# Wider joins of solved blocks, a router written as rows, and more filler products in the routing

## The chip, the cores and the metric

The kernel runs on one core of a Trainium2 chip. The metric is the device time of one execution in microseconds. All data is fp32. The engines are TensorE (PE: matmul, and its weight loads, PEld), VectorE (DVE), ScalarE (ACT), GpSimd (POOL) and SyncE (SP, which here only issues DMAs).

## What is computed

A recurrence over 768 steps for 4 x 8 heads of width 40, and two mixtures of experts on its output, each of which sends a token to one of 8 experts.

```python
for t in range(S):                                   # S = 768
    y[:, :, t] = einsum('bhd,bhde->bhe', rt, state)
    Sa = einsum('bhde,bhe->bhd', state, at)
    state = state * wt[:, :, None, :] - einsum('bhd,bhe->bhde', Sa, bt) \
            + einsum('bhd,bhe->bhde', vt, kt)
x = y as (3072 tokens, 320)
# layer 1: e = argmax(x @ w_gate); out = softmax weight * sigmoid(x @ w_output_gate)[e] * relu(x @ w1[e]) @ w2[e]
# layer 2: the same without the output gate, on layer 1's output, with a capacity of 768 tokens per expert
```

w1[e] is 320 x 1024 and w2[e] 1024 x 320.

## The kernel before

**The recurrence.** Time is cut into chunks of 64 steps (C) and the work into 12 sets (NK): a set k is 128 steps (two chunks, c = 0 and 1) of 16 heads, so 32 pieces, 16 on each side h of the partitions (rows 0 to 63 and 64 to 127). Within a chunk the steps depend on each other through a lower triangle of 64 x 64 (a Gram matrix of a and b, `G_b`), which has to be solved: T = (1 - G)^-1. It is solved in blocks. Four diagonal blocks of 16 (BLK) are solved by DVE in `solve`, all heads at once, on rows that go out to DRAM and come back in another layout (`send_g`, `fetch_g`; `send_t`, `fetch_t`, `fetch_d`). Then PE joins them: two blocks of 16 to one of 32 by `join_first` (G times T, to `A_sb`) and `join_second` (D_nat^T times A_sb, to T_T through `t16_out`), for both halves m of the chunk; then two blocks of 32 to 64 by `quotient` and `corner`.

**The order.** Each engine has its program, and all are built from one loop over slots j = -3 to 12, with two halves c = 0, 1 each. In slot j the chain of the state runs for set j (`right_side`, `state_natural`, `solved`, `state`, `inner`, `outputs`), the solving for set j + 1 and `grams_b` for set j + 2. On PE the half c = 1 has `right_side`, `grams_b(j+2)`, `state_natural`, `natural`, `outputs`, `join_first(j+1)`, `turn_y`, `solved`, `state`, `grams_k`, `join_second(j+1)`, `inner`, `quotient(j+1)`. The half c = 0 has `right_side`, `grams_k`, `corner`, `state_natural`, `outputs`, `natural`, `solved`, `state`, `inner`. DVE's `m_out` (line 1277) masks what `inner` made and so ends each half; after the one of c = 1 DVE does `solve(j+2)`, on which POOL's `scale_a` and `scale_run` wait, and on these PE's next `grams_b` (line 856).

**Lines.** A product is one call of `mm`; in the trace an fp32 product is two matmuls and two weight loads. `join_first` is line 909, `join_second` 924, `quotient` 938, `corner` 955, `right_side` 969, `state_natural` 986, `grams_k` 875, `solved` 997 and 1005, `inner` 1037 and 1041, `outputs` 1054 and 1062, `turn_y` 1073. ACT's copies all have line 665: `gb_out` (G_b), `ga_out` (A_sb), `t16_out` (T_T), `u_out` (ZV). POOL: `scale_a` 575, `scale_run` 582, `mask_gk` 589.

**The second router.** In slot 2 ACT's queue issues one DMA (line 761) that writes the second router's weights, 320 x 8, transposed into DRAM (`wr_dram`). Before the experts begin, SP's queue spreads them over all partitions (`wr_next`, line 540).

**The routing**, once per layer: a chain of small DVE operations on [128, 24 x 8]; PE counts tokens with two products (1128), then does WARM products of 128 x 128 by 512 whose result nobody reads (1132), then 24 products (1136) that sort tokens and gates into 31 tiles, in four lots, each after one of four DVE operations of line 1419 (`place_set`). After it DVE hands the tokens to POOL, which gathers rows by indirect DMA.

**The experts**: 31 tiles of 128 tokens per layer. PE: `up(i+1)` (1160, 1167), `turn_x(i+2)` (1147), `down(i)` (1179). ACT and DVE: relu (816, 1444). DVE: `result` (1451) and, in the first layer, `next_logits`, a multiplication of `wr_next` by the tile's rows (1458) and a sum (1462). DVE's order per tile is relu of i + 1, result of i, logits of i; POOL stores the tile (646) after its logits. `lg_parts` holds partial logits of the first router between `x_out` on ACT and `lg_sum` on DVE.

## Time and profile before

| | us |
|---|---|
| median of 3 runs | 1289.96 (1289.43 to 1297.5) |
| the profiled execution | 1287.04 |
| its span | 1285.3 |

| engine | busy us | share |
|---|---|---|
| PE | 1097.9 | 85% |
| PE weight loads | 949.7 | 74% |
| DVE | 558.7 | 43% |
| ACT | 396.4 | 31% |
| POOL | 302.4 | 24% |

The busy times come from the page, which also has the chain of work that ended last, followed back from the last instruction. The mean granted clock of PE over the whole span is 0.876 of full speed. In what follows a "stretch" is a piece of time between two given points, in us from the start of the span. "issue" is time in which an engine waited for nothing that the profile shows.

### The profile page before, as it was taken

Reading aid. Unit: us, or ns where it says so; the run is one execution under the profiler, and the core shown is the slowest. Engines: PE = TensorE matmul, PEld = TensorE weight load, DVE = VectorE, ACT = ScalarE, POOL = GpSimd, SP = SyncE. Lnnn points to the kernel's source line nnn. Section 1 sums busy time; section 2 is a strip of 40 time slices with the busy share of each in tenths; the row PEclk is TensorE's granted clock in tenths of the full one; section 3 lists DMA queues with packets and bytes.
Section 4 is the critical chain, followed back from the end, with each engine's and each line's share of the span. In section 5 each row is a group of like instructions: output and inputs, shape, how many; then the busy total and the mean of one; then the engine's idle time right before and its main releaser. Section 6 shows DMA issues by size and latency. Waiting matters only on the chain.

```text
span 1285.3 us, 41335 instructions
## 1 busy us (share of the span) xinstructions
PE 1097.9 (85%) x18328; PEld 949.7 (74%) x18328; DVE 558.7 (43%) x864; ACT 396.4 (31%) x550; POOL 302.4 (24%) x253
## 2 busy tenths in 40 slices
PE   1189894888898889986899999999569999997997
PEld 0188784777888878885788888888448888876885
DVE  6635363364536443416176777767650111110111
ACT  0033332333333334331333333333004333323330
POOL 5440443043034213000112122121201212121111
PEclk8557997896888689777799999999868999998999
DMA  3333439343334333216024224333300331443000
GB/s 84 93 96 84 101 88 68 78 95 81 95 74 110 81 88 74 56 40 199 18 74 146 66 77 129 98 115 103 87 7 29 123 107 61 141 139 112 21 11 1
DMA packets 143115, 107.64 MB, mean 84 GB/s; under 512 B 91553, under 2 KB 120233, under 8 KB 142813
## 3 DMA queue, kind: packets, MB, share of 16 engines
q1 hardware_dynamic: 130560, 84.99, 25.0%
q0 software_dynamic: 6016, 16.05, 3.9%
q10 hardware_dynamic: 6364, 3.96, 2.0%
q8 instruction: 148, 2.42, 0.8%
q14 instruction: 27, 0.21, 0.1%
HBM read 87.51 MB, written 22.09 MB: 85 GB/s over the span
## 4 chain that ended last, share of the span: by engine, by line
PE 76%; DVE 8%; issue 7%; POOL 3%; DMA 3%; ACT 2%; SPq 1%; ACTq 0%; POOLq 0%; DVEq 0%
PE pair L1179 19%; PE pair L1160 17%; PE pair L1167 5%; PE pair L986 4%; PE bank L1054 3%; PE pair L1147 2%; PE pair L875 2%; PE pair L1073 2%; POOL AG L575 2%; PE bank L969 2%; PE bank L1062 2%; PE pair L892 2%; PE pair L924 2%; PE bank L1136 2%; PE pair L909 2%
## 5 line engine op out<-in xcount | busy, mean ns | idle before, releaser
L1179 PE MATMUL pair<-abk_own,H_nat 128*128 x992 | 277.7, 433 | 1.7 <-DVE S_nat L1451 1.7
L1160 PEld LDWEIGHTS pair<-H_nat,rvm 128*128 128x128 f32 x1984 | 238.3, 197 | 23.0 <-ACT H_nat L665 14.2
L1160 PE MATMUL pair<-H_nat,rvm 128*128 128x128 f32 x1984 | 239.6, 281 | 11.9 <-ACT H_nat L665 11.9
L1179 PEld LDWEIGHTS pair<-abk_own,H_nat 128*128 128x128 f32 x992 | 183.9, 190 | 71.3 <-issue 2.7
L665 ACT ACTIVATE rvm<-ring_own 128x2560 f32 x62 | 145.0, 2339 | 149.5 <-issue 86.0
L816 ACT ACTIVATE H_nat<-pair 128x512 f32<-128x512 f32 x62 | 37.0, 596 | 289.4 <-PE pair L1167 289.4
L1451 DVE TENSOR_SCALAR S_nat<-pair,gate_all 128x320 f32<-128x320 f32 x62 | 34.1, 551 | 206.1 <-PE pair L1179 206.1
L1444 DVE TENSOR_SCALAR H_nat<-pair 128x512 f32<-128x512 f32 x62 | 42.5, 686 | 167.0 <-PE pair L1167 167.0
L575 POOL TENSOR_TENSOR AG<-abk_own,F_run 40x512 f32<-40x512 f32 x48 | 60.3, 1257 | 173.9 <-DVE T_nat L1254 143.5
L589 POOL TENSOR_SCALAR_AFFINE_SELECT AG<-AG 64x512 f32<-64x512 f32 x48 | 43.1, 899 | 202.6 <-ACT AG L665 200.2
L646 POOL DMA_INDIRECT between<-S_nat,token_all x31 | 33.9, 1094 | 234.7 <-DVE S_nat L1462 226.6
L646 POOL DMA_INDIRECT out<-S_nat,token_all x31 | 31.5, 1016 | 244.7 <-DVE S_nat L1451 236.7
L1458 DVE TENSOR_TENSOR AG<-AG,S_nat 128x2560 f32<-128x2560 f32 x31 | 87.6, 2825 | 1.1
L1462 DVE TENSOR_REDUCE S_nat<-AG 128x8 f32<-128x2560 f32 x31 | 87.4, 2820 | 1.1
L1271 DVE TENSOR_TENSOR y_T<-bank,F_run 128x512 f32<-128x512 f32 x24 | 16.6, 691 | 131.3 <-PE pair L1073 77.6
L1167 PE MATMUL pair<-H_nat,rvm 64*128 64x128 f32 x992 | 72.1, 285 | 0.0
L1167 PEld LDWEIGHTS pair<-H_nat,rvm 64*128 64x128 f32 x992 | 60.2, 187 | 7.5
L986 PE MATMUL pair<-table_sb,ring_own 128*128 128x104 f32 x384 | 61.2, 325 | 4.4 <-issue 4.4
L665 ACT ACTIVATE H_nat<-pair 128x384 f32<-128x384 f32 (+1 forms) x86 | 47.0, 546 | 51.3 <-PE pair L892 50.5
L986 PEld LDWEIGHTS pair<-table_sb,ring_own 128*128 128x128 f32 x384 | 56.4, 233 | 6.0 <-issue 4.6
L582 POOL TENSOR_TENSOR abk_own<-abk_own,E_run 128x1024 f32<-128x1024 f32 x24 | 57.9, 2413 | 1.9
L636 POOL DMA_INDIRECT y_T<-x_dram,token_all x31 | 31.8, 1027 | 76.8 <-DVE tile_i L1437 67.3
(137 smaller groups left out, 1501.2 us busy)
## 6 DMA issues: line engine op xcount, KB each, us to landing
abk_own<-w SPq DMA_DIRECT2D x16, 1280.0 KB, 8.6
ring_own<-w SPq DMA_DIRECT2D x16, 512.0 KB, 3.6
ring_own<-w SPq DMA_DIRECT2D x32, 256.0 KB, 4.6
t_dram<-T_rows SPq DMA_DIRECT2D x12, 384.0 KB, 2.4
ring_own<-w SPq DMA_DIRECT2D x32, 128.0 KB, 5.2
w_in<-wT SPq DMA_DIRECT2D x48, 80.0 KB
abk_own<-aT SPq DMA_DIRECT2D x24, 160.0 KB
abk_own<-bT SPq DMA_DIRECT2D x24, 160.0 KB
```

The lines of the kernel that those rows point to most:

```text
L575: nc.gpsimd.tensor_tensor(heads(AG[q, u % 5, o]), heads(a_in[q, :, :, c * C:(c + 1) * C]), fruns(k)[q, c::CC, 0:C], ALU.mult).then_inc(a_s ...
L582: nc.gpsimd.tensor_tensor(runs, runs, E_run[:, k % 2, 2:].rearrange("p (n t) -> p n t", t=C + 1)[:, :, 0:C], ALU.mult).then_inc(signal, 1)
L589: return nc.gpsimd.affine_select(t, t, [[0, t.shape[1]], [1, C]], ALU.is_gt, 0.0, base=0, channel_multiplier=-1)
L646: pool.indirect_dma_start(out=result_of[s], out_offset=bass.IndirectOffsetOnAxis(ap=token_all[:, s, i:i + 1], axis=0), in_=y_rows[i % 2][: ...
L665: nc.scalar.activation(dst, src, ACT.Copy, scale=scale).then_inc(signal, 1)
L986: last = mm(pair[0][:, b, a * P:a * P + SPAN], Z_diag[:, diag_of(u), b * NPAIR + a, :], ident[:, 0:SPAN], start=True, stop=True)
L1160: mm(to, w1_now[:, par, k * F + m * P:k * F + m * P + P], xT[:, (0, 2 - m // 4)[k], :], start=(m % 4 == 0 and k == 0), stop=False, skip_gr ...
L1167: last = mm(view(2 * par + half, 4, P)[:, m, :], w1_now[q, par, at:at + P], xT[q, 1 + half, :], start=False, stop=True, skip_group_check=True)
L1179: last = mm(bank[5][:, 0:DM], hidT[par][:, k, :], ring2[:, bass.ds(place, 1), k, :].rearrange("p a d -> p (a d)"), start=(k == 0), stop=(k ...
L1444: v.tensor_scalar(hidT[par][:, 4:8, :], view(2 * par + 1, 4, P), 0.0, None, ALU.max).then_inc(L["h_relu_dve"][s], 1)
L1458: v.tensor_tensor(terms, wr_next[:, :, :], y_rows[i % 2][:, 0:DM].unsqueeze(1).to_broadcast([P, E, DM]), ALU.mult).then_inc(terms_made, 1)
L1462: v.tensor_reduce(y_rows[i % 2][:, DM:ROW], terms, AX_X, ALU.add).then_inc(lg_made, 1)
```

## The change

- Both joins do two blocks of 16 at once. `join_first` takes all 64 rows of a side with weights of 64 columns and a moving operand of 2 x 16 columns (before: 32 rows, 16 columns, 16 moving, once per half m). `join_second` takes 64 rows, a 64-column `D_nat` and 32 moving columns (before: 16, 16, 16). 32 products each per set in place of 64. Products of blocks that don't belong together come out too, and are either not read or multiplied by zero.
- For that `D_nat` becomes block diagonal and is cleared once by POOL; `A_sb` is twice as wide; and POOL zeroes the upper right 32 x 32 of each G_b (`cut_g`, two memsets per set, after ACT's copy), for which `join_first` waits.
- The second router's weights are written as the 320 rows of 8 that they are, and `next_logits` reads them through a rearranged view.
- WARM goes from 6 to 11 products per layer.
- `lg_parts` is a ring of two sets instead of a place for each, with a wait.

```diff
 AHEAD = 3
-WARM = 6
+WARM = 11
 BLK = 16
...
         T_nat = sb("T_nat", [P, 2, BLK, BLK])
-        D_nat = sb("D_nat", [P, CC * H, BLK])
-        A_sb = sb("A_sb", [P, CC * H, BLK])
+        D_nat = sb("D_nat", [P, CC * H, C])
+        A_sb = sb("A_sb", [P, CC * H, 2, BLK])
         products = sb("products", [P, BLK, BLK])
...
         lg_all = sb("lg_all", [P, NG, 2 * E])
-        lg_parts = sb("lg_parts", [P, NG, NPAIR, 2 * E])
+        lg_parts = sb("lg_parts", [P, 2, 2, NPAIR, 2 * E])
...
         ring2 = part(abk_own, 0, 2, FC, DM)
-        terms, wr_next = [part(AG[:, :, :, :, :, :].rearrange("p u o b a t -> p (u o b a t)"), n * E * DM, E, DM)
-                          for n in range(2)]
+        A_flat = AG[:, :, :, :, :, :].rearrange("p u o b a t -> p (u o b a t)")
+        terms = part(A_flat, 0, E, DM)
+        wr_next = part(A_flat, E * DM, DM, E)
         w1_now = part(rvm[:, :, :, :, :].rearrange("p n b a t -> p (n b a t)"), 0, 2, W1_COLS)
...
         tn_dram = nc.dram_tensor("tn_dram", [2, 2, NBLK, CC * H, BLK, BLK], F32, kind="Internal").ap()
-        wr_dram = nc.dram_tensor("wr_dram", [E, DM], F32, kind="Internal").ap()
+        wr_dram = nc.dram_tensor("wr_dram", [DM, E], F32, kind="Internal").ap()
         x_dram = nc.dram_tensor("x_dram", [N, DM], F32, kind="Internal").ap()
...
         z_cleared = sem("z_cleared")
+        g_cut = sem("g_cut")
+        d_cleared = sem("d_cleared")
         m_ready = sem("m_ready")
...
                     if n % 2 == 0:
-                        sp.dma_start(D_nat[rows_of(h, n), :, :],
+                        sp.dma_start(D_nat[rows_of(h, n), :, n * BLK:(n + 1) * BLK],
                                      tn_dram[k % 2, h, n].rearrange("x t s -> t x s")
...
                         sp.wait_ge(t16_ready, solve_set)
+                    else:
+                        sp.wait_ge(d_cleared, 1)
                     fetch_d(solve_set)
...
             sp.wait_ge(wr_turned, 16)
-            sp.dma_start(wr_next, wr_dram.unsqueeze(0).to_broadcast([P, E, DM])).then_inc(wr_landed, 16)
+            sp.dma_start(wr_next, wr_dram.unsqueeze(0).to_broadcast([P, DM, E])).then_inc(wr_landed, 16)
...
             nc.gpsimd.memset(Z_diag, 0.0).then_inc(z_cleared, 1)
+            nc.gpsimd.memset(D_nat[:, :], 0.0).then_inc(d_cleared, 1)
             pool.wait_ge(cleared, CLEARS)
...
+            def cut_g(k):
...
+                pool.wait_ge(gb_copied, k + 1)
+                for h in range(2):
+                    nc.gpsimd.memset(G_b[SIDE[h]:SIDE[h] + HALF, k % 2].rearrange("p c o a t -> p (c o a) t")[:, :, HALF:C],
+                                     0.0).then_inc(g_cut, 1)
+                    pool.wait_ge(g_cut, 2 * k + h + 1)
...
                     mask_gk(2 * nat_set)
+                if grams:
+                    cut_g(gram_set)
+                if nats:
                     mask_gk(2 * nat_set + 1)
...
                 for h in range(2):
-                    copy(A_sb[half_rows(h)].rearrange("p x t -> p (x t)"),
-                         pair[1][half_rows(h), h, 0:CC * H * BLK], ga_copied)
+                    copy(A_sb[half_rows(h)].rearrange("p x m t -> p (x m t)"), pair[1][half_rows(h), h, :], ga_copied)
...
                                  "p u o a t -> p (u o a) t"),
-                             pair[0][q, h, 0:CC * H * BLK].rearrange("p (x t) -> p x t", t=BLK), t16_copied)
+                             pair[0][q, h, :].rearrange("p (x m t) -> p x m t", m=2, t=BLK)[:, :, m, :], t16_copied)
...
                          pair[2][:, b, :].rearrange("p (a o d) -> p a o d", a=NPAIR, o=2)[:, :, :, 0:D], x_copied)
-                copy(lg_parts[:, 2 * s * NT + t:(2 * s + 1) * NT + t + 1:NT],
+                if k >= 2:
+                    act.wait_ge(lg_summed, k - 1)
+                copy(lg_parts[:, k % 2],
                      pair[2][:, :, :].rearrange("p b (a t) -> p b a t", t=P)[:, :, :, D:D + 2 * E], x_copied)
...
-            def turn_router():
-                act.dma_start(wr_dram, router_w[1, :, 0:E].rearrange("d e -> e d"),
-                              allow_slow_non_contiguous=True).then_inc(wr_turned, 16)
+            def load_next_router():
+                act.dma_start(wr_dram, router_w[1, :, 0:E]).then_inc(wr_turned, 16)
...
                     if c == 1 and j == 2:
-                        turn_router()
+                        load_next_router()
...
                 pe.wait_ge(t_landed[k % 2], 16 * T_DMAS * (k // 2 + 1))
+                pe.wait_ge(g_cut, 2 * (k + 1))
                 if k + 1 < NK:
...
                 pe.wait_ge(gk_copied, 2 * (2 * k + 1))
-                for m in range(2):
-                    for c in range(CC):
-                        for a in range(NPAIR):
-                            for o in range(2):
-                                for h in range(2):
-                                    at = (c * H + o * NPAIR + a) * BLK
-                                    q = SIDE[h] + m * HALF
-                                    last = mm(pair[1][q:q + BLK, h, at:at + BLK],
-                                              G_b[q:q + HALF, k % 2, c, o, a, m * HALF:m * HALF + BLK],
-                                              T_T[q:q + HALF, (2 * k + c) % 4, o, a, m * HALF + BLK:(m + 1) * HALF],
-                                              start=True, stop=True)
+                for c in range(CC):
+                    for a in range(NPAIR):
+                        for o in range(2):
+                            for h in range(2):
+                                at = (c * H + o * NPAIR + a) * HALF
+                                q = half_rows(h)
+                                last = mm(pair[1][q, h, at:at + HALF].rearrange("p (m t) -> p m t", m=2),
+                                          G_b[q, k % 2, c, o, a, :],
+                                          T_T[q, (2 * k + c) % 4, o, a, :].rearrange(
+                                              "p (m n t) -> p m n t", m=2, n=2)[:, :, 1, :],
+                                          start=True, stop=True)
                 last.then_inc(ga_ready, 1)
...
                     pe.wait_ge(ut_copied, 2 * k)
-                for m in range(2):
-                    for x in range(CC * H):
-                        for h in range(2):
-                            q = slice(SIDE[h] + m * HALF, SIDE[h] + m * HALF + BLK)
-                            last = mm(pair[0][q, h, x * BLK:(x + 1) * BLK], D_nat[q, x, :], A_sb[q, x, :],
-                                      start=True, stop=True)
+                if k == 0:
+                    pe.wait_ge(d_cleared, 1)
+                for x in range(CC * H):
+                    for h in range(2):
+                        q = half_rows(h)
+                        last = mm(pair[0][q, h, x * HALF:(x + 1) * HALF], D_nat[q, x, :],
+                                  A_sb[q, x, :, :].rearrange("p m t -> p (m t)"), start=True, stop=True)
                 last.then_inc(t16_ready, 1)
...
                 here = slice(2 * s * NT + t, (2 * s + 1) * NT + t + 1, NT)
-                v.tensor_reduce(lg_all[:, here, :], lg_parts[:, here].rearrange("p g a x -> p g x a"),
+                v.tensor_reduce(lg_all[:, here, :], lg_parts[:, k % 2].rearrange("p g a x -> p g x a"),
                                 AX_X, ALU.add).then_inc(lg_summed, 1)
...
                         dve.wait_ge(lg_made, i)
-                    v.tensor_tensor(terms, wr_next[:, :, :],
+                    v.tensor_tensor(terms, wr_next.rearrange("p d e -> p e d"),
                                     y_rows[i % 2][:, 0:DM].unsqueeze(1).to_broadcast([P, E, DM]), ALU.mult
```

## Rows read from the trace of the kernel before

**Rows 1.** The page, its parts 1 and 4: busy times, and the last chain by engine.

```profile
PE 1097.9 (85%) x18328; PEld 949.7 (74%) x18328; DVE 558.7 (43%) x864; ACT 396.4 (31%) x550; POOL 302.4 (24%) x253
...
PE 76%; DVE 8%; issue 7%; POOL 3%; DMA 3%; ACT 2%; SPq 1%; ACTq 0%; POOLq 0%; DVEq 0%
```

**Rows 2.** Busy us by stretch, ten back ones: PE, PEld, DVE, ACT, POOL; clock, DMA, GB/s.

```profile
95.70:118.50 22.80, 20.00 (x729) 17.95 (x727) 9.37 (x13) 8.47 (x16) 2.43 (x4) 0.83 0.46 105
...
405.50:433.40 27.90, 22.21 (x758) 19.78 (x754) 11.47 (x12) 8.78 (x19) 10.17 (x6) 0.85 0.41 102
...
sum 239.00, PE 200.24 PEld 180.29 DVE 97.28 ACT 87.91 POOL 53.67; mean PE 20.02 PEld 18.03 DVE 9.73 ACT 8.79 POOL 5.37
```

**Rows 3.** The same view of eight front stretches.

```profile
389.70:405.50 15.80, 14.90 (x440) 13.58 (x436) 11.46 (x38) 6.99 (x12) 5.39 (x5) 0.86 0.33 82
433.40:453.90 20.50, 19.93 (x450) 18.58 (x451) 11.49 (x39) 6.96 (x12) 9.83 (x8) 0.62 0.29 63
...
sum 144.30, PE 136.75 PEld 126.18 DVE 91.44 ACT 54.52 POOL 59.13; mean PE 17.09 PEld 15.77 DVE 11.43 ACT 6.82 POOL 7.39
```

**Rows 4.** DMA queues, 176.7 to 199.3 us: packets, MB, share of 16 engines.

```profile
q8 instruction: 6, 0.10, 1.7%
```

**Rows 5.** DMA queues, 200 to 218 us.

```profile
q10 hardware_dynamic: 2510, 0.02, 71.2%
```

**Rows 6.** Line 446, the send of solved rows to t_dram, all 12.

```profile
DMA to landing us min/median/max: 2.3/2.4/21.4
```

**Rows 7.** Timeline of PE, 199 to 240 us: start, us, instructions, idle before them.

```profile
210.51 0.95 PE L986 MATMUL pair<-table_sb,ring_own 128*128 128x104 f32 x3 [4.41 <-issue]
...
225.00 1.72 PE L1062 MATMUL bank<-rvm,H_nat 128*40 128x64 f32 x27 [10.36 <-issue]
...
232.01 1.08 PE L1005 MATMUL pair<-T_T,R_sb 64*40 64x64 f32 x28 [2.36 <-issue]
```

**Rows 8.** Timeline of PE, one slot from 376 us.

```profile
391.90 1.97 PE L875 MATMUL pair<-AG,abk_own 64*64 64x64 f32 x32
...
405.22 1.13 PE L969 MATMUL bank<-ZV,AG 128*64 128x40 f32 x32
407.05 1.16 PE L856 MATMUL pair<-abk_own,AG 64*64 64x64 f32 x64 [0.70 <-POOL abk_own L582]
...
413.80 1.69 PE L909 MATMUL pair<-T_T,G_b 32*16 32x16 f32 x128
...
419.06 2.68 PE L1073 MATMUL pair<-table_sb,y_T 128*128 128x104 f32 x11 [2.83 <-issue]
...
425.47 1.15 PE L875 MATMUL pair<-AG,abk_own 64*64 64x64 f32 x32
```

**Rows 9.** Timeline of PE, the first layer's routing.

```profile
597.21 6.18 PE L1132 MATMUL bank<-table_sb 128*128 128x512 f32 x12
607.01 10.50 PE L1136 MATMUL bank<-T_T,F_run 128*128 128x62 f32 x48 [3.61 <-DVE F_run L1419]
```

**Rows 10.** The last chain in order of time, two tiles of the first expert layer.

```profile
640.32 3.57 PE pair L1160 x32
...
649.77 3.57 PE pair L1160 x32
```

**Rows 11.** Groups by line and shape, DVE: busy us, mean ns, idle before.

```profile
L1458 DVE TENSOR_TENSOR AG<-AG,S_nat 128x2560 f32<-128x2560 f32 x31 | 87.6, 2825 | 1.1
L1462 DVE TENSOR_REDUCE S_nat<-AG 128x8 f32<-128x2560 f32 x31 | 87.4, 2820 | 1.1
...
L1444 DVE TENSOR_SCALAR H_nat<-pair 128x512 f32<-128x512 f32 x62 | 42.5, 686 | 167.0 <-PE pair L1167 167.0
...
L1451 DVE TENSOR_SCALAR S_nat<-pair,gate_all 128x320 f32<-128x320 f32 x62 | 34.1, 551 | 206.1 <-PE pair L1179 206.1
...
L1402 DVE TENSOR_TENSOR G_b<-G_b,base 128x192 f32<-128x192 f32 x2 | 0.7, 358 | 0.1
...
L1404 DVE TENSOR_TENSOR G_b<-G_b 128x192 f32<-128x192 f32 x2 | 1.0, 508 | 0.1
```

## The prediction

> **What bounds the kernel now.** I read the page first [rows 1]: TensorE (PE) is busy for 85% of the span and holds 76% of the chain that ended last, so what PE does or waits for is what counts. But 7% of that chain, some 90 us, is "issue", time in which PE waits for nothing that the profile shows. The first half of the span, to about 590 us, is the recurrence; there it has to be looked for.
>
> I then cut the recurrence at the DVE operation of line 1277 (`m_out`), which ends each half of a slot. Ten "back" stretches (from `m_out(2j)` to `m_out(2j+1)`, with `grams_b` and both joins) last 239.0 us together, 23.9 each; PE is busy for 20.0 of that, so 3.9 us of each are gaps; the ten granted clocks go from 0.83 to 1.00, with a mean of 0.90 [rows 2]. Eight "front" stretches, without joins, last 18.0 us on the mean, PE busy 17.1, clock 0.62 to 0.90, mean 0.78 [rows 3]. The ninth, 199.7 to 237.5, is left out of this mean; it is an accident of its own, below.
>
> The gaps have a pattern. In the timeline of PE [rows 8] `turn_y` of 419.06 stands behind a hole of 2.83 us in the middle of one run of equal products: no data can be missing there. What is missing is instructions. PE's stream comes by the instruction queue in packets of 16 KB, 256 instructions of 64 B. The DMA view has 6 of them in 22.6 us of a dense stretch, one per 3.8 us [rows 4]. A product of fp32 is two weight loads and two matmuls, 4 instructions. A back stretch has 378 products, so 1512 instructions or 5.9 packets: at 3.8 us each that is 22.4 us, nearly the whole 23.9. A front stretch has 210 products, 3.3 packets, 12.5 us of 18.0. So the back stretches live at the pace of the instruction supply, and the joins, whose 128 matmuls pass in 1.69 us [rows 8], eat one packet of supply in less than half the time that it takes to come.
>
> **The accident at 199.7 us.** `turn_router` writes the second router's weights transposed, one element at a time: 320 x 8 = 2560 packets of 4 B. From 200 to 218 us ACT's queue q10 has 2510 packets and takes 71.2% of 16 engines' time [rows 5]; no row of the instruction queue stands in that answer. The send of the solved blocks takes 21.4 us where the median is 2.4 [rows 6], and PE has holes of 4.41, 10.36 and 2.36 us, all "issue" [rows 7].
>
> **The change, part by part**, on the profiled execution's own time, 1287.0 us (span 1285.3 plus 1.7), 3 under the median of 1290.0.
>
> *Router as rows.* 320 packets of 32 B replace 2560 of 4 B. Holes of 17.1 us go, less the 2.8 us that such a stretch has anyway (below): **-14**. Bounds: -10 if an eighth of the packets still holds the queue for an eighth of the time (2 us) and the next stretches give some back; -18 if the cold clock behind the holes goes too.
>
> *What it costs later.* `wr_next` now holds [320, 8], and `next_logits` reads it with a step of 8 floats. The trace has that very step: L1404 and L1402 are the same multiplication or addition of 192 elements, L1404 with one operand stepping by 8 floats: 508 against 358 ns [rows 11]. 150/192 = 0.78 ns more per element; over 2560 elements L1458 goes from 2825 to 4824 ns. Is it hidden? In the first expert layer DVE needs 0.69 + 0.55 + 4.82 + 2.82 = 8.9 us per tile, about 9.1 with issue [rows 11]; PE needs 9.45 per tile (640.32 to 649.77) [rows 10]. PE stays the bound, by 0.35 us. At the layer's end it is not covered: the last two tiles' logits stand in one line on DVE ahead of the last store, so 2 x 2.0 = **+4**. Lower bound 0 (no penalty as operand 0), upper bound: if the step doubles the whole time, to 5.6 us, DVE takes over (rival C).
>
> *WARM 6 to 11, twice.* Six products, 12 matmuls, take 6.18 us, the first ones cold; PE then idles for 3.61 us on DVE's one-hot (L1419), the clock falls, and 48 matmuls of L1136 run cold in 10.50 us, 219 ns each [rows 9]. Five more products are 10 matmuls of 512 columns at the warm 0.43 us (6.18 less two cold at 0.86, over 10): 4.3 us, which fills the 3.6 and overshoots by 0.7. If the clock holds, L1136 goes at the pace of the nearest warm row, 3.57 us for 32 matmuls with 128 columns of weights, 112 ns [rows 10]: 5.4 us. DVE feeds its four lots in 3.6 us, so it doesn't bind. -5.1 + 0.7 = -4.4, twice: **-9**. If the clock doesn't hold: +1.4.
>
> *Wider joins.* Each join goes from 64 products to 32, that is 64 matmuls of 64 weight columns by 32. Nearest warm rows: L875 (64 columns by 64, also two quarters of the array) 32 in 1.15 us with its tail, 34 ns each to the next; L969 (64 by 40) 1.13 [rows 8]. The moving width hardly matters, so I take 34 ns: 64 x 34 = 2.18 us against 1.65 now, +0.53, two per set, 12 sets: **+13**. Lower bound 17 ns, -14; upper bound the cold L875, 1.97 us for 32 [rows 8], 59 ns.
>
> *One packet less.* 64 products fewer per set are 256 instructions, one packet of 9.2. A back stretch then needs 4.9 packets, 18.7 us: less than PE's own work. Of the 3.9 us of gaps some 1.1 wait for ACT and POOL; of the 2.8 for instructions I take 2.2 as gone, for 11.5 sets: **-25**. Bounds 0 and -32.
>
> *Clock.* The stretches with joins and holes are followed by cold ones: 0.85, then 0.62 over 433.4 to 453.9, where PE is busy for 19.93 of 20.5 us [rows 2, 3]. In the cold L875 takes 1.97 us for 1.15 [rows 8]. A clock of 0.90 is 20% of 23.9 us cold, worth 2.4; in the front 0.78 is 44% of 18.0, worth 4.0, of which 2.2 at most can be had, for the fastest stretch of its kind (15.8 us, [rows 3]) already meets POOL: PE waits 0.70 us for `b_scaled` [rows 8]. Fewer holes and products that fill 64 x 64 cells instead of 16 x 16 should keep some of it: I take 1.7 of 4.6 us per set, 11 sets: **-19**. Bounds 0 and -45.
>
> *Costed at nothing.* `cut_g` on POOL (two fills of 512 elements) stands between the two `mask_gk`, where POOL waits for ACT anyway; the second mask is needed only half a slot later. Without that cover it is some 1.2 us per set. Queued behind its wait for `gb_copied` is only that second mask, whose own wait ends later. A_sb's two copies double to 512 columns, +0.2 us each, while PE runs `turn_y` and `solved`; behind them ACT has `u_out`, which PE needs after `solved`, over 3 us later. `D_nat`'s fill lies before PE's start, under DVE's fills. `lg_parts` as a ring waits for a sum a whole slot old.
>
> Sum: -14 + 4 - 9 + 13 - 25 - 19 = -50; 1287 - 50 = 1237 of span and rest, 1240 on the median; I write 1241.
>
> The Trainium skill speaks against two of these terms. Its page "Runtime: NRT & Kernel Launch", section "Instruction fetch mechanics", has the same 16 KiB blocks of 256 instructions, but calls the cost of crossing one mostly hidden. By it the -25 would be nothing and the time 1266, which is rival A with the clock's share kept; the holes inside runs of equal products and the 5.9 packets per 23.9 us say otherwise. Its page "TensorE: Matmul & The Clock Gate", section "LDWEIGHTS", gives a load as its columns over 1.2 GHz: 53 ns for 64, and the joins would cost +42 instead of +13; the 34 ns of L875 and L969 deny it.
>
> **The rivals.**
> A. *The joins give nothing*: the supply is late elsewhere instead, the clock falls as before. For it: holes stand also in `inner` and `quotient` (L1037, L938), behind the joins. Against: the back stretch's demand falls below its work. The supply term halves to -12, the clock's is nothing: 1290 - 14 + 4 - 9 + 13 - 12 = 1272.
> B. *WARM doesn't hold the clock*: L1136 is no dense work, 10.5 us of it don't raise the clock today [rows 9]. Then +1.4 in place of -9: 1251.
> C. *DVE becomes the bound in the first expert layer*: it decides from 5.2 us for L1458 on. At a plain doubling (5.6 us) DVE needs 9.9 per tile, +0.45 x 31 = +14, and 1.6 more at the tail: 1257. Against: at L1404's extra per element it is 4.8 us, 1.9 ns per element and not 2.2.
> D. *Slower*: the wide products run cold. At 59 ns a join is 3.8 us, +2.1, 24 times +51; with the supply's and the clock's gains lost: 1290 - 14 + 4 - 9 + 51 = 1322. It decides from 38 ns per matmul on, where 24 joins cost the 19 us that the other terms bring. Against: at both places the clock is up today when the joins begin (L875 beside the second join takes its warm 1.15 us, [rows 8]).
>
> **How the numbers follow.** Forecast 0.62 (own range 1226 to 1258), A 0.15, B 0.08, C 0.08, D 0.04, and 0.03 for the better bounds of joins and clock together (under 1222). The range 1222 to 1274 takes in the forecast, B, C and A's centre, about 0.85. About 1%, 13 us, is what a measurement of this kernel can tell from no change: faster by more (under 1277) 0.91, within 0.05, slower 0.04.
>
> **What would show it.** Right: period at j = 2 like its neighbours and t_dram's landing maximum near 2.4; 12 instruction packets fewer; back stretches near 21.5 us with gaps under 2; the wide matmuls at 34 ns; L1136 in about 5.5 us per layer; L1458 at 4.8 us with PE's tile still 9.45. Wrong: packets gone but gaps unchanged (A); tile period above 9.45 (C); join runs of over 3 us (D).

## The result, and the profile after

The kernel became slower, by 3%, where I had forecast 4% faster.

| | before | after |
|---|---|---|
| median, us | 1289.7 (1288.81 to 1297.5, 4 runs) | 1331.59 (1329.18 to 1334.18, 4 runs) |
| ratio | | 1.031 (1.027 to 1.036) |
| profiled execution, its span | 1287.04, 1285.3 | 1334.18, 1332.4 |

In the kernel after, line numbers stand 3 to 19 higher: `join_first` 926, `join_second` 943, `grams_b` 873, `inner` 1056 and 1060, WARM 1151, the routing's 24 products 1155, `turn_x` 1166, `up` 1179 and 1186, `down` 1198, `m_out` 1296; on DVE `next_logits` 1477 and 1481 and `result` 1470; on POOL `scale_run` 588, the gather of rows 653 and the store 663.

I read the two traces by stage first. The stages are cut at two DVE operations of each routing, the one that completes the choice of the expert (line 1360, after 1379) and the last one (1437, after 1456), and at the end:

| stage | before, us | after, us | difference | forecast |
|---|---|---|---|---|
| recurrence, up to the first routing | 595.2 | 555.0 | -40.2 | -45 |
| routing, layer 1 | 22.9 | 19.4 | -3.5 | -4.4 |
| experts of layer 1 | 319.4 | 412.7 | **+93.3** | +4 |
| routing, layer 2 | 24.1 | 19.2 | -4.9 | -4.4 |
| the rest | 323.7 | 326.1 | +2.4 | 0 |

So four of five stages did nearly what the sum said (in the recurrence by errors that cancel, see below), and in one, where I had costed the strided read at 4 us, 93 were lost. Which wait carries it is in the view of waits of the kernel after, PE alone (who waited for whom; us in total, times, longest):

```profile
PE pair L1166 <- DMA y_T<-x_dram,token_all: 60.7, 15, 6.9
PE pair L873 <- POOL abk_own L588: 51.4, 5, 23.7
```

Before, PE lost 4.1 us in the first row's place, in one wait at the start of the layer, which every kernel here has. Of the second row 23.7 and 9.7 us lie at the very start of the recurrence, as before; its other three waits come up below. What PE waits for in the first row are the rows of x that POOL gathers by indirect DMA for the tile after next. The groups of the kernel after, with busy us and mean ns, show what became late:

```profile
L1477 DVE TENSOR_TENSOR AG<-AG,S_nat 128x2560 f32<-128x2560 f32 x31 | 149.5, 4821 | 1.1
...
L653 POOL DMA_INDIRECT y_T<-x_dram,token_all x31 | 92.0, 2967 | 64.0 <-DVE tile_i L1456 54.5
```

The multiplication takes 4.82 us, as worked out (4.824, from [rows 11]). But POOL's instruction that prepares the gather, which doesn't touch the router, went from a mean of 1027 to 2967 ns. One tile in the timelines of DVE, POOL and PE (start, us) shows how:

```profile
708.98 0.55 DVE L1470 TENSOR_SCALAR S_nat<-pair,gate_all 128x320 f32<-128x320 f32 x1 [0.59 <-PE pair L1198]
709.57 4.81 DVE L1477 TENSOR_TENSOR AG<-AG,S_nat 128x2560 f32<-128x2560 f32 x1
```

```profile
708.59 1.02 POOL L663 DMA_INDIRECT between<-S_nat,token_all  x1 [12.57 <-DVE S_nat L1481]
709.91 5.33 POOL L653 DMA_INDIRECT y_T<-x_dram,token_all  x1 [0.31 <-issue]
718.02 1.02 POOL L663 DMA_INDIRECT between<-S_nat,token_all  x1 [2.79 <-DVE S_nat L1481]
719.35 1.02 POOL L653 DMA_INDIRECT y_T<-x_dram,token_all  x1 [0.31 <-issue]
```

```profile
712.45 1.16 PE L1186 MATMUL pair<-H_nat,rvm 64*128 64x128 f32 x16
717.23 0.55 PE L1166 MATMUL pair<-table_sb,y_T 128*128 128x128 f32 x3 [3.62 <-DMA y_T<-x_dram,token_all]
```

The gather starts 0.34 us into the multiplication and ends 0.86 us after its end (715.24 against 714.38). The next one, at 719.35, meets no multiplication and takes 1.02. Of the 31 gathers of the layer 14 last 5.3 us, all of them started inside a run of L1477, and the 14 tiles that wait for such a gather's rows take 14.6 to 18.7 us from one `up` to the next; the 17 others last 1.0 to 1.2, and the tiles between take 9.45. The late one delays PE, so DVE idles, so the next gather is free: every second one is hit.

In the kernel before, a tile of that stage had the store's preparation at 704.11; the timelines of POOL and DVE go on:

```profile
705.43 1.02 POOL L636 DMA_INDIRECT y_T<-x_dram,token_all  x1 [0.31 <-issue]
```

```profile
707.09 2.82 DVE L1458 TENSOR_TENSOR AG<-AG,S_nat 128x2560 f32<-128x2560 f32 x1
```

The gather ended 0.64 us before the multiplication began and had started 1.66 us before it. The multiplication's growth of 2.0 us pushes the store, and the gather behind it, 2.0 us back: 0.34 us past the start of the next multiplication, which is what the trace after shows. The growth came out of DVE's idle time, and DVE's idle time was where POOL did its work.

The windows of this stage give the two parts of the 93.3 us. Before, in 319.4 us, PE is busy for 295.9 and the granted clock is 0.96. After (stretch, us, busy us of PE, PEld, DVE, ACT, POOL, clock, DMA share, GB/s):

```profile
574.40:987.10 412.70, 328.44 (x2077) 264.99 (x2077) 274.50 (x131) 104.82 (x94) 129.27 (x63) 0.88 0.23 71
```

PE's idle time grew by 60.7 us (84.3 less 23.5), 56.6 of it in the first row of the waits (60.7 less 4.1), and its busy time for the same 2077 matmuls by 32.6. After the holes the granted clock is lower: 1.00 in 704.5 to 714.0, 0.82 in the 9.6 us that follow. The two means of the clock, 0.96 and 0.88, account for some 27 of the 32.6 (an estimate, 295.9 x 0.965 / 0.885); I don't explain the rest.

### The profile page after: what moved, and what is told of

Read it like the earlier page. It is cut to its first block, busy times and chain, and to the rows that moved or that the text cites. A ratio compares the mean times of both kernels' runs of the same rounds, so it can differ in the third digit from the quotient of the medians.

```text
span 1332.4 us, 38352 instructions
## 1 busy us (share of the span) xinstructions
PE 1104.9 (83%) x16812; PEld 942.0 (71%) x16812; DVE 624.8 (47%) x864; ACT 403.1 (30%) x550; POOL 387.6 (29%) x278
## 3 DMA queue, kind: packets, MB, share of 16 engines
q1 hardware_dynamic: 130560, 84.99, 23.5%
## 4 chain that ended last, share of the span: by engine, by line
PE 58%; DVE 17%; DMA 11%; issue 5%; POOL 4%; ACT 3%; SPq 1%; ACTq 0%; POOLq 0%; DVEq 0%
PE pair L1198 17%; PE pair L1179 10%; DMA y_T<-x_dram,token_all 8%; DVE AG L1477 6%; PE pair L1005 4%; DVE S_nat L1481 3%; PE bank L1073 3%; PE pair L1186 3%; POOL AG L581 2%; PE pair L1166 2%; PE pair L926 2%; PE pair L1092 2%; PE bank L1081 2%; PE pair L943 2%; PE pair L909 2%
## 5 line engine op out<-in xcount | busy, mean ns | idle before, releaser
L1198 PE MATMUL pair<-abk_own,H_nat 128*128 x992 | 303.1, 462 | 3.2 <-DVE S_nat L1470 1.7
L1198 PEld LDWEIGHTS pair<-abk_own,H_nat 128*128 128x128 f32 x992 | 197.8, 205 | 87.5 <-issue 25.5
L1179 PE MATMUL pair<-H_nat,rvm 128*128 128x128 f32 x1984 | 241.3, 282 | 13.6 <-ACT H_nat L682 13.6
L1477 DVE TENSOR_TENSOR AG<-AG,S_nat 128x2560 f32<-128x2560 f32 x31 | 149.5, 4821 | 1.1
L663 POOL DMA_INDIRECT between<-S_nat,token_all x31 | 35.8, 1155 | 267.4 <-DVE S_nat L1481 259.3
L653 POOL DMA_INDIRECT y_T<-x_dram,token_all x31 | 92.0, 2967 | 64.0 <-DVE tile_i L1456 54.5
L1166 PE MATMUL pair<-table_sb,y_T 128*128 128x128 f32 x186 | 37.9, 318 | 64.7 <-DMA y_T<-x_dram,token_all 60.7
L1166 PEld LDWEIGHTS pair<-table_sb,y_T 128*128 128x128 f32 x186 | 21.3, 153 | 73.1 <-DMA y_T<-x_dram,token_all 59.3
L1290 DVE TENSOR_TENSOR y_T<-bank,F_run 128x512 f32<-128x512 f32 x24 | 16.6, 691 | 114.1 <-PE pair L1092 89.0
L588 POOL TENSOR_TENSOR abk_own<-abk_own,E_run 128x1024 f32<-128x1024 f32 x24 | 65.7, 2739 | 1.9
```

Of the source, the lines that this page charges most:

```text
L588: nc.gpsimd.tensor_tensor(runs, runs, E_run[:, k % 2, 2:].rearrange("p (n t) -> p n t", t=C + 1)[:, :, 0:C], ALU.mult).then_inc(signal, 1)
L653: pool.indirect_dma_start(out=x_rows[i % AHEAD][:, 0:(DM, ROW)[s]], out_offset=None, in_=source_of[s], in_offset=bass.IndirectOffsetOnAxis ...
L663: pool.indirect_dma_start(out=result_of[s], out_offset=bass.IndirectOffsetOnAxis(ap=token_all[:, s, i:i + 1], axis=0), in_=y_rows[i % 2][: ...
L1166: last = nc.tensor.transpose(view(4, 3, P)[:, k, :], x_rows[i % AHEAD][:, at:at + P], ident)
L1179: mm(to, w1_now[:, par, k * F + m * P:k * F + m * P + P], xT[:, (0, 2 - m // 4)[k], :], start=(m % 4 == 0 and k == 0), stop=False, skip_gr ...
L1198: last = mm(bank[5][:, 0:DM], hidT[par][:, k, :], ring2[:, bass.ds(place, 1), k, :].rearrange("p a d -> p (a d)"), start=(k == 0), stop=(k ...
```

## The experiments

The ratio of each is to the kernel before, timed on the same chip in the same job. The kernel before itself has medians of 1278, 1288 and 1282 us in the three jobs, so kernels of different jobs are compared by their ratios.

| kernel | us | ratio to before |
|---|---|---|
| e1_turned | 1242.06 | 0.973 (0.964 to 0.981) |
| e2_ahead4 | 1243.02 | 0.972 (0.964 to 0.980) |
| e3_rows_only | 1356.8 | 1.062 (1.048 to 1.076) |
| e4_joins_only | 1264.94 | 0.989 (0.982 to 0.996) |
| e5_two | 1275.46 | 0.995 (0.990 to 0.999) |
| e6_one | 1273.15 | 0.989 (0.985 to 0.993) |
| e7_late_decays | 1231.2 | 0.956 (0.951 to 0.962) |
| e8_narrow_back | 1297.37 | 1.008 (1.004 to 1.012) |
| e9_warm6 | 1249.85 | 0.976 (0.972 to 0.981) |
| e10_router_only | 1267.95 | 0.986 (0.981 to 0.992) |

### Is it the strided read: turn the router once on the chip

The theory: the longer multiplication locks POOL's gather out. The rival: the loss comes from something else of the change, or DVE is simply the bound. `e1_turned` is the kernel after, but ACT turns the 320 x 8 weights once, 2560 elements, before the experts:

```diff
+        wr_rows = part(A_flat, 0, DM, E)
-        wr_next = part(A_flat, E * DM, DM, E)
+        wr_next = part(A_flat, E * DM, E, DM)
...
+                    act.wait_ge(wr_landed, 16)
+                    copy(wr_next, wr_rows.rearrange("p d e -> p e d"), wr_set)
...
-                    v.tensor_tensor(terms, wr_next.rearrange("p d e -> p e d"),
+                    v.tensor_tensor(terms, wr_next[:, :, :],
```

> The changed kernel with one edit: the router's rows of 8 are turned once on the chip, by one ScalarE copy of 2560 elements during the first routing, so that each tile's logits multiplication reads its weights without a step. Everything else of the change stays. Theory 1 (the multiplication of 4.82 us pushes the store of a tile back by 2 us, and the gather that follows it then falls on the next multiplication, during which GpSimd can't prepare it): the multiplication is 2.8 us again, every gather 1.02 us, no wait of TensorE for the gather, tile period 9.45 us in the first expert layer, that layer shorter by about 93 us, total 1238 to 1245. Rival 2 (the first expert layer lost its 93 us to something else of the change, the clock or the code of the wider joins, or the weights' transfer as rows): the layer stays near 390 us and the total near 1330.

Measured: ratio 0.973, span 1236.2 us. In e1_turned PE's wait is back at its old size, and so are the gathers (of line 655: durations in ns, least, median, most):

```profile
PE pair L1170 <- DMA y_T<-x_dram,token_all: 4.1, 1, 4.1
```

```profile
L655 POOL DMA_INDIRECT y_T<-x_dram,token_all x31: 1000/1024/1203, 570.9 to 847.5; - x31
```

One copy of 2560 elements turns the change from 3% slower to 3% faster. The strided read is the cause.

### Is DVE the bound, or is the gather late: one more buffer

`e2_ahead4` keeps the strided read of 4.8 us and gathers four tiles ahead instead of three:

```diff
-AHEAD = 3
+AHEAD = 4
...
+        x_own = sb("x_own", [P, ROW])
-        x_rows = [y_flat[:, n * ROW:(n + 1) * ROW] for n in range(AHEAD)]
+        x_rows = [y_flat[:, n * ROW:(n + 1) * ROW] for n in range(AHEAD - 1)] + [x_own[:, :]]
```

> The changed kernel, with its stepped multiplication of 4.82 us, but gathers run four tiles ahead instead of three (a fourth buffer for gathered rows). VectorE has exactly the same work. Theory 1 (the gather is late): gathers may still last 3 to 5.3 us each, but TensorE no longer waits for them, the tile period is 9.45 us and the total 1240 to 1250, 4 us of it the longer tail of two stepped multiplications. Rival 3 (VectorE itself is the bound with 8.9 us and its waits per tile, and the waits for the gather only show it): the period stays as in the changed kernel, 9.45 and 15 to 18 us in turn, total near 1330.

Measured: ratio 0.972, the same as with the turned router, and DVE works as long as in the kernel after. Groups on POOL, then PE's wait, which is the same row as in e1_turned:

```profile
L657 POOL DMA_INDIRECT y_T<-x_dram,token_all x24 | 110.9, 4620 | 65.9 <-DVE tile_i L1460 58.8 <-issue 7.0
...
L657 POOL DMA_INDIRECT x_own<-x_dram,token_all x7 | 32.9, 4703 | 2.1 <-issue 2.1
```

```profile
PE pair L1170 <- DMA y_T<-x_dram,token_all: 4.1, 1, 4.1
```

26 of the 31 gathers are now locked out (at 702.34 for 5.31 us, at 711.77 for 5.34), and PE doesn't care, because they have a tile more of time; its tile is 9.45 us again. So DVE with 9.1 us per tile is not the bound, as the prediction said; being locked out costs nothing by itself; being late does.

### The two parts alone

`e3_rows_only` is the kernel before with only the router written and read as rows:

```diff
-                act.dma_start(wr_dram, router_w[1, :, 0:E].rearrange("d e -> e d"),
-                              allow_slow_non_contiguous=True).then_inc(wr_turned, 16)
+                act.dma_start(wr_dram, router_w[1, :, 0:E]).then_inc(wr_turned, 16)
...
-                    v.tensor_tensor(terms, wr_next[:, :, :],
+                    v.tensor_tensor(terms, wr_next.rearrange("p d e -> p e d"),
```

> The kernel before with one part of the change: the second router written as rows and read with a step of 8 floats; narrow joins and 6 filler products. Theory 1: the recurrence loses the stall at 200 us, 14 to 20 us (the period there 42 us instead of 59), the first expert layer gains 90 to 95 us, total 1360 to 1370. Rival 2: the total falls by 14 to 20 us, to about 1272, since what cost the layer came with the other parts.

Measured: 1356.8 us (two runs, 1347 and 1367), ratio 1.062, the slowest of all: the loss without the gains. In its trace the recurrence is 13.6 us shorter than before, and the first expert layer again has 14 gathers of 5.3 us. PE's waits:

```profile
PE pair L1147 <- DMA y_T<-x_dram,token_all: 60.2, 15, 6.6
```

`e4_joins_only` is the kernel after with the router and WARM of before, so only the wider joins are new:

```diff
-WARM = 11
+WARM = 6
...
-        wr_dram = nc.dram_tensor("wr_dram", [DM, E], F32, kind="Internal").ap()
+        wr_dram = nc.dram_tensor("wr_dram", [E, DM], F32, kind="Internal").ap()
```

> The kernel before with the wider joins alone (and the smaller ring of partial logits); the router is transposed element by element as before, 6 filler products. The prediction's terms for the joins were +13 for the products, -25 for the instruction supply, -19 for the clock: -31, total 1259. From the changed kernel's trace I now expect less, -15 to -20 (total 1270 to 1275), since in its first sets TensorE gains 5 us per set and gives it back waiting 6 us for GpSimd's scaling. If the wider products were no gain at all: 1290.

Measured: ratio 0.989 (0.982 to 0.996), -13.5 us; in its own trace the recurrence is 21.5 us shorter than before (573.7 against 595.2). The prediction had -31 for this part (13 - 25 - 19), so by the ratio about a half came; I had by then expected -15 to -20, which the -13.5 just misses. The accident of the element-wise router is still there and has moved onto PE as one single hole; PE's timeline of e4_joins_only:

```profile
208.35 0.31 PE L1081 MATMUL bank<-rvm,H_nat 128*40 128x64 f32 x3
226.87 1.44 PE L1081 MATMUL bank<-rvm,H_nat 128*40 128x64 f32 x23 [18.21 <-issue]
```

No data can be missing between two products of one run, and the trace has no instruction packet between the one that ends at 200.9 and the one that begins at 224.0 us, where those before came mostly 4 to 5 us apart. Into that time fall 2547 packets of 4 B on ACT's queue q10. The kernel before has such a gap of 17.8 us in the same place; in the kernels that write the router as rows (after, e1, e3, e7, e8, e10) no gap after 100 us in the recurrence is over 11.7 us. This is the clearest view in this case of the 2560 element writes keeping the instruction queue from its turn.

`e10_router_only` is the kernel before with the router as rows and turned by ACT, joins and WARM as before (its diff is that of e3 and e1 together).

> The kernel before with nothing changed but the second router's weights: moved as rows and turned once on the chip by ScalarE, so that VectorE's multiply reads without a stride; joins and warming products as before. The prediction put the moved router at -14 us, all of it from the one slow front stretch of the recurrence (37.8 us where the others have 11.8 to 16). The trace of the kernel after has the whole recurrence 40 us shorter, and the joins alone measured -13.5 us, so if the parts add up the router is worth -22 to -27 us (ratio 0.979 to 0.983). If -14 is right the ratio is 0.989. The gathers should last 1.03 us each, and VectorE's multiply 2.82 us.

Measured: ratio 0.986 (0.981 to 0.992), so -17.7 us. The interval holds the 0.989 of the prediction's -14 and also the 0.983 at the low end of the other expectation, so it doesn't decide between them; -14, with its bounds of -10 and -18, stands unrefuted. In its own trace (of an execution 11 us above its median) the recurrence is 9.9 us shorter than before, and "issue" in it 16.6 (38.6 for 55.2).

`e9_warm6` is e1_turned with `WARM = 6`.

> The kernel after with the router turned once on the chip (as in e1_turned), but with 6 warming products per routing chain as before instead of 11. By the prediction's term (48 products of L1136 in 5.5 instead of 10.5 us, 4.4 us per layer, two layers) it is some 8 us slower than e1_turned: a ratio to the kernel before of about 0.979 where e1_turned measured 0.973, the 48 routing products at 10.5 us again in both layers, and the stretch from the first row of the last block to the first expert layer 3.5 to 5 us longer in each. If the extra products do not carry the time (the rival that they only fill time that is waited for anyway), the ratio stays at 0.973 and the 48 products stay near 5.5 us.

Measured: ratio 0.976 (0.972 to 0.981), 0.0036 above e1_turned, with intervals that overlap, so the time alone doesn't settle it. The traces do: from the choice of the expert to the first gather it takes 21.5 and 24.3 us with six products, 18.6 and 19.8 with eleven, 7.4 us less for both layers. The 48 matmuls behind them take 8.9 and 10.5 us with six, 5.5 and 5.5 with eleven.

### What locks POOL out: two operands, or just lateness

`e5_two` and `e6_one` are e1_turned (contiguous multiplication, 2.82 us) with one more DVE instruction of 1.99 us per tile ahead of it, whose result nobody reads: in e5_two a product of two SBUF operands, in e6_one a sum of one.

```diff
+                    v.tensor_tensor(extra_to[:, :], extra_in[:, :], extra_by[:, :], ALU.mult).then_inc(extra_done, 1)
```

```diff
+                    v.tensor_reduce(extra_to[:, 0:EXTRA // 8], extra_in[:, :].rearrange("p (a b) -> p a b", b=8), AX_X, ALU.add).then_inc(extra_done, 1)
```

> The kernel with the router turned on the chip (e1_turned), and 2 us more VectorE work per tile of the first expert layer, ahead of the logits multiplication: a multiplication of two SBUF operands, 1760 elements, 1.99 us, without a step, whose result nobody reads. VectorE's time per tile is then that of the changed kernel. Theory 1 (a gather isn't prepared while VectorE runs an operation that reads two operands from SBUF; the step matters only by the time it takes): the gather after each late store falls on this multiplication and the next, 4.8 us together, lasts about 5 us again, TensorE waits at every second tile, total 1320 to 1335. Rival 4 (it is the step of 32 bytes itself that keeps GpSimd out): gathers stay near 1.0 us, total 1246 to 1250.

> As e5_two, but the 2 us are a sum that reads one SBUF operand (1760 elements in groups of 8). VectorE's time per tile is the same. Theory 1: the late gather is issued while this sum runs, takes 1.0 us and is on time; tile period 9.45 us, total 1246 to 1250 (the 4 us are the longer tail). Rival 5 (the time alone matters: a store that is 2 us later is enough): total 1320 to 1335 as e5_two.

Both missed on the time. In e5_two the lock is there but short (13 gathers of 2.6 to 2.8 us); the timelines of DVE and POOL:

```profile
692.68 1.99 DVE L1486 TENSOR_TENSOR F_run<-T_T 128x1760 f32<-128x1760 f32 x1
694.59 2.82 DVE L1487 TENSOR_TENSOR AG<-AG,S_nat 128x2560 f32<-128x2560 f32 x1
```

```profile
692.92 2.65 POOL L659 DMA_INDIRECT y_T<-x_dram,token_all  x1 [0.31 <-issue]
```

The gather starts 0.24 us into the first product and is through at 695.57, 0.90 us after that product's end, although the second product has been running since 694.59. I had expected it to be held over both, to 698. It is one instruction that locks POOL out, not busy time: at the boundary between two it gets in. 4.8 us in one piece is worse than 2.0 and 2.8 in two, for the gather; the loss isn't gone, for the ratio is 2.2% above e1_turned's.

In e6_one the gather is issued during the one-operand sum and isn't held at all:

```profile
691.30 1.99 DVE L1486 TENSOR_REDUCE F_run<-T_T 128x220 f32<-128x1760 f32 x1
```

```profile
691.54 1.03 POOL L659 DMA_INDIRECT y_T<-x_dram,token_all  x1 [0.31 <-issue]
```

So a product of two SBUF operands locks POOL out without any stride, and the stride only made the instruction long; a sum of one operand doesn't lock it out. The two added instructions differ also in kind, multiplication and reduction, which no run here separates from the number of operands. Still e6_one is 1.6% slower than e1_turned by the ratios, where I had expected nearly nothing, and in the traces its first expert layer is 32.5 us longer. PE waits for gathered rows 21.0 us in 8 tiles, 4.1 of it in the one that every kernel has. None of the gathers is held on POOL (1.0 to 1.2 us each). Behind the one at 700.99 the rows land 6.2 us after the instruction's end where the median is 1.9, and SP's queue issued the next expert's weights at 700.15; 1.8 MB move on that queue until the rows have landed. 7 gathers of e6_one land over 4 us after their instruction's end, as many as there are new waits. In e1_turned, where the gather starts 2 us earlier, none does for which the trace has the landing (at most 3.6 us), and only the common tile waits. So the second mechanism here is plain lateness: a gather that starts 2 us later has no spare left for the tiles in which weights are being loaded. e5_two has both in its 25.0 us of waits, and I can't divide them.

### A second lock in the recurrence, and the best version

After shows three back stretches of 28.4 to 32.5 us where the others take 20.5 to 22.3 (stretch, us, PE, PEld, DVE, ACT, POOL, clock, DMA, GB/s):

```profile
129.40:161.90 32.50, 25.11 (x642) 23.28 (x639) 12.14 (x13) 10.57 (x21) 13.89 (x10) 0.79 0.36 85
174.80:203.70 28.90, 21.59 (x643) 19.94 (x640) 12.09 (x12) 10.53 (x21) 13.90 (x10) 0.88 0.40 95
...
303.40:325.40 22.00, 20.39 (x642) 18.51 (x640) 9.79 (x13) 10.58 (x21) 8.83 (x7) 1.00 0.44 112
...
sum 239.20, PE 204.50 PEld 187.59 DVE 100.94 ACT 103.96 POOL 86.80; mean PE 20.45 PEld 18.76 DVE 10.09 ACT 10.40 POOL 8.68
```

Each holds one wait of PE for POOL, and POOL is slow there beside DVE's scan, which has two SBUF operands; the timelines of PE, POOL and DVE:

```profile
181.10 1.99 PE L873 MATMUL pair<-abk_own,AG 64*64 64x64 f32 x64 [5.94 <-POOL abk_own L588]
```

```profile
176.98 8.30 POOL L588 TENSOR_TENSOR abk_own<-abk_own,E_run 128x1024 f32<-128x1024 f32 x2
```

```profile
175.94 3.15 DVE L1242 TENSOR_TENSOR_SCAN E_run<-w_in,ones_at 128x1041 f32<-128x1041 f32 x1
...
181.00 2.31 DVE L1251 TENSOR_TENSOR_SCAN F_run<-w_in,start_at 128x1040 f32<-128x1040 f32 x1
```

Two `scale_run` take 8.30 us; the median of one is 2.19. Each overlaps one scan. It works the other way too: the first scan starts while POOL's `scale_a` still runs, to 176.91, and takes 3.15 us where the second has 2.31. `e7_late_decays` is e1_turned with these scans moved behind `y_out` on DVE, off the moment in which POOL scales:

```diff
-                if loads:
-                    decays(j + 3)
                 if chain:
                     y_out(2 * j)
+                if loads:
+                    decays(j + 3)
```

> e1_turned with one edit in the recurrence: VectorE's decay scans for the set after next (two scans of 2.3 and 2.6 us that read two SBUF operands) come after the masking of the outputs of the same half instead of before it, so that they start some 8 us later and not while GpSimd scales b and k. In the changed kernel the first sets have GpSimd's two scalings at 4.1 us instead of 2.2 each beside these scans, and TensorE waits 6 us for them. Theory: these waits shrink to about 2 us in three sets, -6 to -12 us, total 1230 to 1236. Rival: TensorE or the later scans hold the next half up, and the gain is within 3 us or a loss.

Measured: 1231.2 us, ratio 0.956 (0.951 to 0.962), the best version, faster than both kernels. e1_turned's interval (0.964 to 0.981) just doesn't touch it, and the two ran in different jobs. How much the edit brought is less sure: -6.8 us between the two spans (1229.4 for 1236.2), inside the -6 to -12 expected, but over 20 by the ratios. The groups of `scale_run` in e7_late_decays, then in e1_turned:

```profile
L590 POOL TENSOR_TENSOR abk_own<-abk_own,E_run 128x1024 f32<-128x1024 f32 x24 | 54.1, 2255 | 1.9
```

```profile
L590 POOL TENSOR_TENSOR abk_own<-abk_own,E_run 128x1024 f32<-128x1024 f32 x24 | 61.9, 2579 | 1.9
```

POOL is nearly undisturbed now. The recurrence is 5.1 us shorter than in e1_turned (547.2 against 552.3); PE's waits for POOL in it are more in number and shorter (14.9 us, most 4.1, against 11.8, most 6.0), and PE's busy time is 5.2 us less at a clock of 0.91 instead of 0.89. So the gain comes through the clock after shorter holes, as far as the trace tells, not through less waiting.

### Is it the instruction supply: narrow products put back

`e8_narrow_back` is e1_turned with 64 products of 16 x 16 x 16 per set ahead of the wide first join, which overwrites their result.

```diff
+                for m in range(2):
+                    for x in range(CC * H):
+                        for h in range(2):
+                            q = slice(SIDE[h] + m * HALF, SIDE[h] + m * HALF + BLK)
+                            mm(pair[1][q, h, x * BLK:(x + 1) * BLK], T_T[q, 2 * k % 4, 0, 0, 0:BLK],
+                               T_T[q, 2 * k % 4, 0, 0, BLK:2 * BLK], start=True, stop=True)
```

> e1_turned, and ahead of each first join the 64 narrow products of 16 x 16 x 16 that both joins lost together are put back, as work without use (the wide join overwrites what they write). The products cost 128 matmuls at 13 ns, 1.7 us per set, 20 us in all. Theory (the joins' gain is one packet of instructions less per set): the back stretches are again at the pace of the supply, 22.4 us and more, the holes inside runs of equal products come back, and the cost is 35 to 45 us, total 1277 to 1287. Rival (the gain is the clock, held by wide products, which are all still there): the cost is the products' own 20 us or less, total at most 1262.

Measured: ratio 1.008, some 3.6% slower than e1_turned. By the ratios the cost is some 46 us where I had expected 35 to 45, and the rival's 20 or less is out. The instruction packets are back at 148. At the join itself the holes of before are back too; groups of e8_narrow_back (busy us, mean ns, idle before):

```profile
L936 PE MATMUL pair<-T_T,G_b 64*64 64x32 f32 x768 | 32.7, 246 | 5.0 <-issue 5.0
...
L928 PE MATMUL pair<-T_T 16*16 16x16 f32 x1536 | 21.7, 173 | 5.1 <-issue 4.3 <-DMA T_T<-t_dram 0.7
```

9.3 us of "issue" before the first join, where before had 9.5 at the same place and e1_turned none. But over the whole recurrence "issue" is only 17.5 us: 1.5 more than e1_turned's 16.0 with 12 packets fewer, and 21 less than the 38.6 of e10_router_only, which has the same 148 packets and no accident either. So PE has holes where the narrow products stand, but the number of packets doesn't set the sum. The expected way, stretches at the pace of the supply, isn't what cost the time. The recurrence became 63.5 us longer: 47.7 of PE's busy time, of which the new products are 19.7 and the rest goes with the clock (0.85 for 0.89), and 15.8 idle, nearly all of it for POOL.

## Why the prediction was wrong

**Where it failed.** The step is the one that ends "PE stays the bound, by 0.35 us". It asked whether 2 us more on DVE are hidden, and answered by comparing DVE's sum per tile with PE's. Both numbers were right: L1477 took 4.82 us, and where nothing was late PE's tile took 9.45 (e2_ahead4). What it left out is who else uses the time in which DVE is idle. Rival C looked at the same two sums and had the same gap; its threshold, 5.2 us, was not the one that decided. What decided was where the gather came to start. From 0.64 us of growth on it meets the multiplication, from 1.66 us on it starts behind the multiplication's start; the growth was 2.0. What a growth between the two would cost, no run shows. No part of the prediction has POOL's gather in that stage.

**The trace of before had the sign.** The store at the end of the last tile of layer 1 begins 0.27 us into a multiplication. POOL's and DVE's timelines of the kernel before:

```profile
921.15 3.41 POOL L646 DMA_INDIRECT between<-S_nat,token_all  x1 [8.13 <-DVE S_nat L1451]
```

```profile
920.88 2.82 DVE L1458 TENSOR_TENSOR AG<-AG,S_nat 128x2560 f32<-128x2560 f32 x1
```

3.41 us for an instruction that otherwise takes 1.02, and it ends 0.86 us after the multiplication. In the groups this is only a mean of 1094 where the layer-2 twin has 1016. Another sign was `scale_run`, whose 24 have a median of 2.18 us and a maximum of 4.09.

The Trainium skill has the rule. Its page "SBUF — State Buffer", section "SBUF: two separate sides", says that DVE and GpSimd share a pair of SBUF ports which is locked for a whole instruction, by a DVE instruction with two SBUF inputs against a GpSimd one that reads SBUF, and that whoever starts first keeps the other out. The traces agree as far as they go: the gather is out 0.86 to 0.90 us after multiplications of 4.81 and 1.99 us, isn't held beside the one-operand sum, gets in at the boundary of two instructions, and the scan that found `scale_a` running took 0.84 us more. That it matters whether the GpSimd instruction reads SBUF, no run here tests. The prediction didn't weigh this rule.

**Term by term.**

| term | forecast | shown |
|---|---|---|
| router as rows | -14 | -17.7 (interval some 7 either way), e10_router_only; -9.9 and -13.6 in the recurrence of e10's and e3's traces |
| strided read | +4 | +93, stage of the trace; e1_turned against after |
| WARM | -9 | -8.4 in the traces before to after, -7.4 e9 to e1 |
| wide products' own time | +13 | +9.5 of busy time, 5.9 of it from 100 us on |
| instruction supply | -25 | about 0: -25 of "issue", +26 of other waits |
| clock of the recurrence | -19 | some -30 of busy time |

*Router.* The send to t_dram landed after up to 21.4 us [rows 6]; in the kernel after nothing that writes or reads t_dram takes more than 4.3, and the front stretch of 37.8 us takes 13.0.

*Wider joins.* Their groups after, against 21.4 and 21.7 us before:

```profile
L926 PE MATMUL pair<-T_T,G_b 64*64 64x32 f32 x768 | 26.4, 226 | 1.4 <-DMA T_T<-t_dram 1.4
...
L943 PE MATMUL pair<-A_sb,D_nat 64*64 64x32 f32 x768 | 26.2, 226 | 0.4 <-ACT U_T L682 0.4
```

A run of 64 passes in 2.06 us, 32 ns each, where I took 34 from L875 [rows 8]. Rival D is out, but for the first set (3.61 us, cold).

*Supply.* Exactly 12 packets fewer, 136 for 148, as written. The sums of PE's waits in the recurrence (from 100 us to the routing), taken from the view of waits by cause:

| waited for | before | after | e4_joins_only |
|---|---|---|---|
| issue | 55.2 | 13.0 | 30.9 |
| POOL | 3.2 | 17.9 | 22.3 |
| ACT | 11.0 | 19.0 | 19.3 |
| DVE and DMA | 1.4 | 4.5 | 4.4 |

Issue fell by 42.2. 17.1 of that is the accident, and 25.1 are left, the forecast's 25. But 25.8 came back as waits for POOL, ACT, DVE and DMA, so the term is worth nothing in sum, and this is the second step that failed. The likely reason is that PE reached its next inputs sooner and found them not ready; it is argued, not shown, for 14.7 of the 25.8 are waits for POOL in stretches where POOL was also slowed by the scan. For it speaks e7_late_decays, where the scaling is nearly undisturbed and PE still waits 14.9 us for POOL. The prediction wrote "1.1 wait for ACT and POOL" per stretch as if it were a constant. In e4_joins_only the exchange is the same (24.3 less of issue with the accident still in it, 30.4 more of the others). The Trainium skill's page "Runtime: NRT & Kernel Launch", section "Instruction fetch mechanics", calls the cost of a new block mostly hidden. The traces don't decide against it: 25.1 us of "issue" went together with 12 blocks, but e8_narrow_back, with the 12 blocks back, has only 1.5 us more than e1_turned. That the block was the cause, as the prediction had it, is not shown, and the match of 25 with 25 is luck as far as these runs tell.

*Clock.* Granted 0.89 for 0.82 over the recurrence from 100 us on. PE's busy time fell by 23.7 there (420.7 to 397.1) although the joins added 5.9, so the clock gave some 30, more than the 19 taken. Adding up: 30 - 6 of busy time and 16.5 of idle time make the 40.2 us. That the forecast for the stage, -45, came so near is partly luck: the supply's 25 us, which brought nothing in sum, are made up by the clock (11 more), the joins' own time (7 less) and the accident (3 more).

**Right.** WARM, but for a slip in its sum (4.46 us over 10 matmuls are 0.45 us each, not 0.43): 48 matmuls pass in 5.47 us where 10.50 stood [rows 9], so rival B is out; PE's timeline of the kernel after:

```profile
557.02 11.45 PE L1151 MATMUL bank<-table_sb 128*128 128x512 f32 x22
568.30 5.47 PE L1155 MATMUL bank<-T_T,F_run 128*128 128x62 f32 x48
```

Rival A (the joins give nothing) is refuted by e4_joins_only's interval, which ends at 0.996, but its reason, "the supply is late elsewhere instead", was half true, with POOL in place of the supply. The forecast without the strided read would have been 1241 less 4, ratio 0.959; e1_turned, which is that kernel plus one copy, measured 0.973 (0.964 to 0.981). By its trace (span 1236.2 for 1285.3) 49 of those 54 us are there, by the timed ratio two thirds. The medians of before differ by 10 us between jobs, and I don't explain that third. On the sign, the 0.91 for "faster" was far too sure: it rested on one stage that I had looked at closely, while the stage with the fewest questions asked held the loss.

**Open.** How the 25.0 us of e5_two divide between lock and lateness; why e8_narrow_back's new products cost the clock that much; what the "issue" holes before the change were due to, if not to the number of packets; and whether POOL's longer work in the recurrence after (the mean of `scale_run` 2739 ns for 2413) is only chance of alignment, for each kernel has its own.

## What to carry to other kernels

When a DVE instruction with two SBUF operands grows, don't ask only whether DVE still has less to do than the bound. Lay POOL's instructions beside it in the timeline, take the time from the start and from the end of POOL's to the start of DVE's, and compare the growth with that: here 2.0 us against 1.66 and 0.64. A gather that is prepared on GpSimd wants a buffer more, or a layout turned once ahead of the loop; either won back the whole loss here. The same 2 us more as a separate instruction (e5_two) held the gather for less time, but still cost some 2%.

When holes of one kind go, count what the next inputs' owners have spare before booking them as gain: here 25 us of holes less stood beside 26 us of other waits more.

## What the runs showed of the hardware that I had not expected

- A GpSimd instruction that prepares an indirect DMA (1.02 us alone) started inside a DVE instruction with two SBUF operands ends 0.84 to 0.90 us after that instruction, whether it lasts 1.99, 2.82 or 4.81 us; beside a one-operand sum it takes 1.03.
- It is let in at the boundary between two DVE instructions, though the next follows without a gap (e5_two).
- POOL's own multiplication goes from 2.18 to 4.1 us beside DVE's scan.
- While some 2560 DMA packets of 4 B ran, no instruction packet came for 23 us, and PE stood for 18.2 us in the middle of a run of equal products (e4_joins_only).
- Products of 64 x 64 with 32 moving columns, alternating between two quarters of the array, pass at 32 ns per matmul; ones of 16 x 16 at 13.
